# Turning the attention result: transposes and a VectorE addition in place of an fp32 product with two stacked identities

## The reference, cut to what matters

```python
# B, H, S, D = 2, 8, 768, 64; 16 clusters
mask = q_assign[:, :, :, None] == k_assign[:, :, None, :]
scores = scale * np.matmul(q, k.transpose(0, 1, 3, 2))
scores = np.where(mask, scores, -1000000000.0)
scores = scores - np.max(scores, axis=-1, keepdims=True)
attn = np.exp(scores)
attn = attn / (np.sum(attn, axis=-1, keepdims=True) + 1e-09)
return np.matmul(attn, v).astype(np.float32)
# then x = attn_out.transpose(0, 2, 1, 3).reshape(B, S, H * D), _moe_ref(x), _moe2_ref(...)
```

## Time and profile before

| | before |
|---|---|
| runs | 797.24, 796.31, 796.67 us; median 796.67 |
| span of the profiled execution, first to last instruction | 795.3 us (about 1.4 us below the median of the runs) |
| granted TensorE clock, mean | 0.998 |
| PE / PEld busy | 746.4 us (94%) / 660.1 us (83%) |
| DVE / ACT / POOL busy | 418.1 us (53%) / 328.9 us (41%) / 251.6 us (32%) |
| 40 to 305 us (attention) alone: PE, DVE, ACT, POOL busy of 265 us | 251.1, 215.9, 205.2, 140.2 us |

### The profile page before, as it was taken

One profiled execution on the slowest core, in us unless ns is written; L12 is line 12 of the kernel. 1 busy time (PEld: TensorE's weight loads), 2 busy tenths in 40 slices (PEclk: granted clock), 3 DMA queues, 4 the chain that ended last, 5 costly groups with the idle time before them and its releaser, 6 DMA issues.

```text
span 795.3 us, 11657 instructions
## 1 busy us (share of the span) xinstructions
PE 746.4 (94%) x4073; PEld 660.1 (83%) x4073; DVE 418.1 (53%) x787; ACT 328.9 (41%) x678; POOL 251.6 (32%) x244
## 2 busy tenths in 40 slices
PE   2899999999999998998999999999999988899998
PEld 1788888888888887998888888888888878898886
DVE  4688788888878888473531132113111148975320
ACT  2677777777777775121110111101110136453321
POOL 6555465566556404001760000000005035551000
PEclk9999999999999999999999999999999999999999
DMA  4223322224342103000320000001004041101011
GB/s 105 67 68 77 90 63 63 63 77 120 84 151 74 43 1 108 1 1 26 108 79 1 0 1 1 0 1 32 23 0 159 1 132 41 41 5 37 26 41 53
DMA packets 20449, 40.93 MB, mean 51 GB/s; under 512 B 2752, under 2 KB 7104, under 8 KB 19904
## 3 DMA queue, kind: packets, MB, share of 16 engines
q1 hardware_dynamic: 17968, 31.62, 14.0%
q0 software_dynamic: 2448, 8.87, 3.3%
HBM read 31.04 MB, written 3.15 MB: 43 GB/s over the span
## 4 chain that ended last, share of the span: by engine, by line
PE 73%; DVE 11%; ACT 8%; issue 6%; POOL 1%; DMA 0%; DVEq 0%; ACTq 0%; SPq 0%; POOLq 0%
PE ps L1162 24%; PE ps L1241 17%; PE ps L1320 8%; PE ps L1306 5%; PE ps L1083 4%; PE ps L1069 4%; PE ps L1057 3%; PE ps L1030 3%; ACT prob L512 2%; PE ps L1058 2%; ACT k L502 2%; DVE row_min L706 2%; ACT pt_h L524 1%; PE ps L1093 1%; ACT q L501 1%
## 5 line engine op out<-in xcount | busy, mean ns | idle before, releaser
L924 DVE SCALAR_TENSOR_TENSOR hid_l<-ps,hid_h 128x512 fp32r<-128x512 f32 x48 | 33.2, 691 | 201.9 <-ACT hid_h L612 201.9
L713 DVE TENSOR_TENSOR pt_l<-ps,pt_h 128x384 fp32r<-128x384 f32 x192 | 102.5, 551 | 47.8 <-ACT pt_h L524 47.5
L612 ACT ACTIVATE hid_h<-ps 128x512 fp32r<-128x512 f32 x48 | 28.7, 598 | 225.4 <-PE ps L1162 225.4
L524 ACT ACTIVATE pt_h<-ps 128x384 fp32r<-128x384 f32 x192 | 84.1, 489 | 49.1 <-PE ps L1069 48.2
L706 DVE TENSOR_REDUCE row_min<-ps 128x1 f32<-128x768 f32 x96 | 90.2, 940 | 6.5 <-PE ps L1058 6.5
L512 ACT ACTIVATE prob<-ps,row_min 128x768 f32<-128x768 f32 x96 | 87.0, 906 | 1.9 <-DVE row_min L706 1.5
L1069 PE MATMUL ps<-cst,prob 128*128 128x128 f32 x576 | 83.7, 283 | 2.8 <-ACT prob L512 2.7
L1057 PE MATMUL ps<-k,q 80*128 80x384 f32 x192 | 75.1, 391 | 3.5 <-ACT k L502 1.5
L1162 PE MATMUL ps<-un_h,w_h 128*128 128x512 f32 x192 | 74.9, 390 | 1.4 <-DVE un_l L918 1.4
L1241 PE MATMUL ps<-w_h,hid_h 128*128 128x512 f32 x192 | 76.0, 396 | 0.0
L1241 PE MATMUL ps<-w_h,hid_l 128*128 128x512 f32 x192 | 75.5, 393 | 0.0
(11 more groups left out here) (138 smaller groups left out, 1592.5 us busy)
## 6 DMA issues: line engine op xcount, KB each, us to landing
stage<-in_moe_w_ch SPq DMA_DIRECT2D x16, 256.0 KB, 3.2
w_raw<-in_moe_w_ch SPq DMA_DIRECT2D x16, 256.0 KB, 2.6
raw_qk<-in_q SPq DMA_DIRECT2D x16, 192.0 KB, 3.1
raw_qk<-in_k SPq DMA_DIRECT2D x16, 192.0 KB, 3.4
raw_v<-in_v SPq DMA_DIRECT2D x16, 192.0 KB, 2.5
q<-q SPq DMA_DIRECT2D x16, 192.0 KB, 2.6
k<-k SPq DMA_DIRECT2D x16, 192.0 KB, 2.6
out<-out_s SPq DMA_DIRECT2D x12, 256.0 KB, 2.0
```

The source lines that it names most:

```text
L524: nc.scalar.activation(pt_h[a][:, R * hf:R * hf + R, (t % R) * P:(t % R + 1) * P], ps[:, 4 + hf, 0:HALF].rearrange("p (j c) -> p j c", j=R ...
L713: nc.vector.tensor_tensor(pt_l[a][part], ps[:, 4 + hf, 0:HALF].rearrange("p (j c) -> p j c", j=R), as_f32(pt_h[a][part]), ALU.subtract).th ...
```

## The change

`fold_o` becomes three transposing matmuls, which write all 128 rows of `o_s` as columns: 384 columns of bank 6 instead of 192. A new DVE instruction, `join_o`, reads these from PSUM, adds each pair of columns 64 apart and writes the 192 sums to the new SBUF tile `joined`; it counts `o_joined`. `store_x` now waits for that and reads `joined` from SBUF instead of PSUM. `values` waits for `o_joined` where it waited for `x_stored`. In `head` of the DVE block, `join_o(n, 0)` stands where `store_x(n, 0)` stood and `store_x(n, 0)` comes one `store_low` later; `join_o(n, 1)` is put ahead of `minimum(m, ..., 5)`, and `store_x(n, 1)` stays behind it. In the last head `join_o` comes ahead of each `store_x`. The constants lose the 64 columns of `fold`.

```diff
@@ vector engine @@
+            def join_o(n, a):
+                dve.wait_ge(fold_ready, AHEAD + 2 * n + a + 1)
+                nc.vector.tensor_reduce(joined[:, a, :, :],
+                                        ps[:, 6, 0:HALF].rearrange("p (r l d) -> p r d l", r=R, l=2),
+                                        axis=AX.X, op=ALU.add).then_inc(o_joined, 1)
+
             def store_x(n, s, a, i):
                 dve.wait_ge(rden_done, 2 * n + a + 1)
-                dve.wait_ge(fold_ready, AHEAD + 2 * n + a + 1)
-                nc.vector.tensor_tensor(x[:, s, R * a:R * a + R, bass.ds(i * D, D)],
-                                        ps[:, 6, 0:R * D].rearrange("p (r d) -> p r d", r=R),
+                dve.wait_ge(o_joined, AHEAD + 2 * n + a + 1)
+                nc.vector.tensor_tensor(x[:, s, R * a:R * a + R, bass.ds(i * D, D)], joined[:, a, :, :],
                                         rden[:, a, :].unsqueeze(2).broadcast_to([P, R, D]),
                                         ALU.mult).then_inc(x_stored, 1)
@@ vector engine, head @@
                 if not prep1:
                     denominator(n, s, 1)
+                    join_o(n, 0)
+                    invert(n, 1)
                     store_x(n, s, 0, i)
-                    invert(n, 1)
                     for m in range(2 * R):
                         pair_low_part(0, m)
+                    join_o(n, 1)
                     store_x(n, s, 1, i)
                     return
...
                 minimum(m, 1 - s, 2)
+                join_o(n, 0)
+                store_low(m, 1, 0)
                 store_x(n, s, 0, i)
-                store_low(m, 1, 0)
                 if prep2:
                     add_dots(n + 2)
...
                 minimum(m, 1 - s, 4)
-                step(m, 1 - s, 3)
+                store_low(m, 3, 0)
+                store_low(m, 3, 1)
+                join_o(n, 1)
+                minimum(m, 1 - s, 5)
                 store_x(n, s, 1, i)
@@ tensor engine @@
                     if not (isinstance(n, int) and 2 * n + a == 0):
-                        pe.wait_ge(x_stored, AHEAD + 2 * n + a)
+                        pe.wait_ge(o_joined, AHEAD + 2 * n + a)
...
                 for r in range(R):
-                    last = nc.tensor.matmul(ps[:, 6, r * D:(r + 1) * D], o_s[:, r * P:(r + 1) * P], fold,
-                                            start=True, stop=True)
+                    last = nc.tensor.transpose(ps[:, 6, r * P:(r + 1) * P], o_s[:, r * P:(r + 1) * P], ident)
```

More of the change, by code:

```diff
@@ L59, in sb @@
             return stack.enter_context(nc.sbuf_tensor(name, [P] + shape, dt))
-        cst = sb(main, "cst", [P + D + C])
+        cst = sb(main, "cst", [P + C])
         ident = cst[:, 0:P]
-        fold = cst[:, P:P + D]
-        first = cst[:, P + D:P + D + C]
+        first = cst[:, P:P + C]
         ln = sb(main, "ln", [B * NT, 11])
@@ L102, in build @@
         row_sum = sb(att, "row_sum", [2 * NT])
+        joined = sb(att, "joined", [2, R, D])
         den = sb(att, "den", [2, R])
@@ L183, in build @@
         x_stored = sem("x_stored")
+        o_joined = sem("o_joined")
         mask_ready = sem("mask_ready")
@@ L677, in _ @@
             dve.sem_inc(x_stored, AHEAD)
+            dve.sem_inc(o_joined, AHEAD)
             dve.wait_ge(cen_rooted, 1)
@@ L1410 @@
     add("chan_tab", channel_table())
-    two = np.concatenate([np.eye(D), np.eye(D)])
-    add("constants", np.concatenate([np.eye(P), two, np.tile(C - np.arange(C), (P, 1))], 1).astype(np.float32))
+    add("constants", np.concatenate([np.eye(P), np.tile(C - np.arange(C), (P, 1))], 1).astype(np.float32))
     args.append(nc.dram_tensor("out_0", (B, S, DM), F32, kind="ExternalOutput").ap())
```

## The result

The changed kernel takes 804.54 us (median of 4 runs, 801.79 to 807.98) against 796.49 (796.22 to 797.24): ratio 1.010, 95% interval 1.008 to 1.012. The forecast was 801.7 with a range of 797.2 to 810, so the sign and the range were right and the size was 3 us short. The profiled execution took 804.68 us, its span is 802.9 us, 7.6 more than before.

A forecast was written before the change was run, and what follows sets the result against it. A head's period was bound by a DVE part (second minimum to masks), an ACT part and a PE part without folds. Terms 0 + 0.4 + 3.2 + 1.4 = 5.0 us took the span to 800.3, time 801.7; range 797.2 to 810.

The forecast's parts named there:

- PE's saving counts for nothing: PE's folds: 0.40 us less for each of 32, 12.8 us, all off the path, costed at 0.
- the very gap that the prediction named: DVE's gap of 0.29 us ahead of `store_low`, the only one from the second minimum to the masks.
- Join in the DVE part: First join of each head, second minimum to masks: costs 0.47 us, mostly regained; 0.4 us in all.
- a sign of being wrong: Attention loop: heads with a period below 17.4 us would show the prediction wrong.
- What `store_x` reads: First store of each looped head: two SBUF inputs make it wait for running POOL instructions, 3.2 us in all.
- The end of attention: Last head: POOL's sums shift, `store_x` waits more, join precedes the store PE needs; 1.4 us.
- Nothing behind it: From the Fourier stage on PE runs without a break and nothing gives the loss back; no further term.
- not 4 to 6: Sign of being right: the first Fourier matmul, at 309.73 before, comes 4 to 6 us later.
- PE's wait for the masks grows to 0.7 us: Sign of being right, every head: PE's wait grows from 0.32 to about 0.7 us, by the fold's saved 0.4.
- The second join costs 0: Second join of each head: the late minimum is wanted only by an exponential ACT reaches after 57.6; cost 0.
- The mask collides as well: Rival: second mask waits about 0.7 us for POOL in 12 heads, 8.4 us, giving 810.1; systematic collisions 0.17.
- No contention: Rival: `store_x`, moving only 192 values, never waits for POOL; 1.8 us, giving 798.5; chance 0.18.

The follow-up runs named there:

- e3: The kernel before with only the first of three products in each fold, two thirds of the queries left out: 796.07 us, ratio 0.998.
- e1: The changed kernel multiplying first from PSUM, then adding the halves by a reduction with one SBUF input: 802.41 us.
- e2: The changed kernel with `store_x(n, 0)` moved behind the masks, directly ahead of `join_o(n, 1)`: 797.62 us, ratio 1.0006.
- e9: The changed kernel with `minimum(m, 5)` ahead of `join_o(n, 1)` instead of behind it: 804.69 us.
- e10: The changed kernel with late `store_x(n, 0)`; last head has the old fold and store, second store ahead of the last two `pair_l`: 796.34 us.
- e6: The changed kernel with `store_x(n, 0)` directly behind `join_o(n, 0)`, ahead of `store_low`: 803.03 us.
- e12: The kernel before; in the last head the second store behind three `pair_l`, ACT's last `o_s` copy ahead of its last two `pair_high_part`: 795.71 us.

## Why the prediction was right in sign and short in size

- **PE's saving counts for nothing**: right to within 0.2 us a head. e3 took more off PE than the change did and gained 0.18 us a head, by the very gap that the prediction named. In the changed kernel three transposes start 0.11 us apart, but what follows them on PE starts 0.45 or 0.54 us after their start in the first fold of a head and 0.71 in the second, against 0.70 to 0.72 before, and PE's busy time fell by only 0.4 us: most of the saving turned into waiting at once. The 12.8 us are an estimate that no trace shows as time gained.
- **Join in the DVE part, 0.4 us**: the cost is real, the sum has the wrong sign. From the second minimum to the masks head 7, undisturbed, has 179.63 - 173.62 = 6.01 us against 5.85 in the earlier trace rows (5.93 to 5.95 in every other head), more than the 0.09 predicted. But in every head the two masks take 0.44 to 0.48 us instead of 0.61 to 0.63, since they come later against POOL's instruction on v, whose end they had waited for. Without the stores' stretching (6.1 us) and `den`, which in head 13 took 0.65 us beside `w_l` (0.32 in the kernel before), the loop would stand at 5.54 - 6.1 - 0.3 = -0.9 us: a small gain where a small loss was predicted. By the prediction's own list this is a sign of being wrong: four of the 13 periods are below 17.4 us (17.33 to 17.39), those of undisturbed heads.
- **What `store_x` reads, 3.2 us: the step that was mis-sized.** The mechanism is shown by e1 and e2 together. It cost 6.1 us instead of 3.2, which is nearly all of the 3 us that the forecast was short. The prediction took POOL's starts from the heads of the kernel before and shifted DVE against them. But POOL's start moves as well: head 0 lost 0.82 instead of 1.09, head 12 nothing instead of 1.01, and heads 2, 3, 5 and 6 more than 1.0 us each. In those the store arrives 1.00 us behind the join's start, 0.06 later than the 0.94 of the sum (0.53 + 0.47, not 0.47 + 0.47), and `w_l` starts at 0.85 to 0.97. For heads 5 and 6 its own working had the store 0.03 and 0.04 us ahead of `w_l`, less than those 0.06. With such gaps the term should have been given as a chance for each head: the 14 starts of POOL were known only to some tenths of a microsecond. That the time fell into the stated range owes something to the range, which left room for half of the heads to collide.
- **The end of attention, 1.4 us**: measured 1.36, of the same parts. POOL's sums start 0.43 us later against the last mask turn, the last `pair_l` 0.69 later, by that shift and the longer waits ahead of it, and join and store in a row add 0.65.
- **Nothing behind it**: wrong by 0.7 us. PE's idling ahead of the Fourier stage grew from 1.30 to 2.90 us, and the granted clock fell earlier. With this and the larger term the first Fourier matmul came 6.9 us later (316.63 against 309.73), not 4 to 6.
- **PE's wait for the masks grows to 0.7 us**: wrong, and in the wrong direction: 0.32 became 0.15 to 0.18 us. The shorter fold brings PE's transposes forward, but these now wait for `pt_l` of a DVE that is late and for `prob` of ACT, ahead of the mask turn. The wait moved up the chain (the changed kernel's waits, 40 to 305 us: total, times, longest; before, PE had waited for `prob` twice, 0.5 us in all):

```profile
PEld ps L1082 <- DVE pt_l L715: 9.2, 17, 1.3
...
PE ps L1082 <- ACT prob L513: 4.0, 15, 0.5
...
PE ps L1053 <- DVE mask_n L754: 2.3, 14, 0.2
```

- **The second join costs 0**: right (e9). **The mask collides as well**: it did not in the changed kernel, where no pair of masks in the loop took longer than before, but it did in one head of e2. **No contention**: excluded by the rows of the store.

## What to carry to other kernels

Before moving an operand from PSUM to SBUF, ask who else works in SBUF at that moment: the saving was 12.8 us by estimate on an engine with slack, the price a store that takes 0.35 or 1.47 us by the tenth of a microsecond at which it arrives. Put such an instruction where its engine idles anyway, and price collisions as a chance per head, since both engines' times move with every edit. What is gained in a loop can be given back at its end: look in the other engines' queues for the copy that stands behind someone else's wait. And when a profile and the median of the runs disagree by a microsecond or two, compare their granted clocks before believing either.

## What was not expected of the hardware

- Size gives no protection: `den`, a TENSOR_SCALAR with a single SBUF input of 3 elements a row, took 1.21 us beside POOL's sums against 0.16 in most heads, while e1's TENSOR_REDUCE with a single SBUF input of 384 kept its 0.55. So it is not only instructions with two SBUF inputs that wait. A store that met `w_l` started, by its usual duration, when POOL's instruction had 0.14 us of its recorded time left: 138.64 + 1.36 - 0.35 = 139.65 against 138.49 + 1.30 = 139.79.
- POOL waits as well. Its sums `pair` last 1.27 to 1.30 us each, but the last one of the kernel before took 1.74 beside a held-up `pair_l`, and two of e10 took 1.74 and 1.70.
- A store directly behind the join that it reads starts 0.76 to 0.78 us after the join's start in the loop (e6, e9) and 0.65 in the heads outside it. A `store_low`, which does not read the sums, starts 0.53 us after the join's start.
- With TensorE idle for 2.9 us (0.55 us of work in the four ahead of the stage) the granted clock was 0.57 in the last two and 0.50 behind; with 0.70 us of work in the last two it was still 1.00, and was 0.60 and 0.55 only during the stage, though TensorE was then always busy. What decides the moment is open: see e2 against e9, and e12, whose clock did not fall here but at 689 us.
